# Two fused MLPs behind a small convolution: the low-part products of the narrow output loaded with 64 instead of 128 weight columns

## The reference

```python
# x: (2, 4096, 192), weight: (8, 7): a causal convolution over 7 taps, softmax over the taps, one set per head
w = softmax(weight)                       # 8 heads, 24 channels each
x = sum_k w[h, k] * x_padded[:, s + k, h, :]
x = x.reshape(8192, 192)
h = x @ moe_w_in                          # 192 -> 2048
x = (h * clip(h + 3, 0, 6) / 6) @ moe_w_out   # 2048 -> 192
h = x @ moe2_w_in
x = where(h > 0, h, exp(min(h, 0)) - 1) @ moe2_w_out
```

## Time and profile before

| | |
|---|---|
| time, median of 3 runs | 1122.45 us (1122.15 to 1123.27) |
| the profiled execution's own time | 1123.27 us |
| its span, first to last instruction | 1121.5 us |
| TensorE matmul / weight load busy | 99% / 82% |
| VectorE / ScalarE / GpSimd busy | 80% / 56% / 4% |
| DMA | 22.50 MB, mean 20 GB/s |

### The profile page before, as it was taken

How to read it: one execution, slowest core, us unless ns; L and a number is a source line. 1 busy time by engine, 2 the same in 40 slices (tenths; PEclk the granted TensorE clock), 3 DMA queues, 4 the chain that set the end, 5 groups by cost and what they waited for, 6 DMA issues and landing times.

```text
span 1121.5 us, 24081 instructions
## 1 busy us (share of the span) xinstructions
PE 1115.1 (99%) x9744; PEld 918.0 (82%) x9744; DVE 900.5 (80%) x963; ACT 632.8 (56%) x684; POOL 40.7 (4%) x36
## 2 busy tenths in 40 slices
PE   9999999999999999999999999999999999999998
PEld 6888888888888888888888888888888888888886
DVE  7897887878888788887878878788787887876776
ACT  7665655546555555555555555465555655546554
POOL 4432000000000000000000000000000000000000
PEclk9999999999999999999999999999999999999999
DMA  4310010100101001010010100001000010000000
GB/s 156 119 36 32 1 34 0 33 0 0 33 0 33 0 0 33 0 33 0 0 33 0 33 0 1 32 0 33 0 28 5 0 33 0 14 1 11 6 2 29
DMA packets 14761, 22.50 MB, mean 20 GB/s; under 512 B 1424, under 2 KB 5520, under 8 KB 14736
## 3 DMA queue, kind: packets, MB, share of 16 engines
q1 hardware_dynamic: 14592, 22.12, 6.2%
q10 hardware_dynamic: 144, 0.01, 0.0%
HBM read 15.83 MB, written 6.29 MB: 20 GB/s over the span
## 4 chain that ended last, share of the span: by engine, by line
PE 99%; ACT 0%; DVE 0%; issue 0%; DVEq 0%; ACTq 0%
PE acc_a L691 31%; PE h_ps L677 31%; PE acc_b L699 20%; PE h_ps L684 16%; PE h_ps L841 0%; PE h_ps L832 0%; PE acc_a L832 0%; PE h_ps L707 0%; PE acc_a L762 0%; DVE hidden L525 0%; PE acc_a L739 0%; ACT hidden L343 0%; PE acc_b L756 0%; PE acc_b L747 0%; PE acc_b L741 0%; PE acc_a L746 0%
## 5 line engine op out<-in xcount | busy, mean ns | idle before, releaser
L353 ACT CAST g_hi<-hidden 128x1024 fp32r<-128x1024 f32 x255 | 268.4, 1053 | 352.7 <-DVE hidden L530 238.2
L534 DVE TENSOR_TENSOR g_lo<-hidden,g_hi 128x1024 fp32r<-128x1024 f32 x255 | 313.1, 1228 | 127.9 <-ACT g_hi L353 127.9
L677 PE MATMUL h_ps<-in_hi_a,win_hi_a 64*128 64x512 f32 x1012 | 390.8, 386 | 0.0
L691 PE MATMUL acc_a<-g_hi,wout_hi_a 64*128 64x512 f32 x1012 | 390.8, 386 | 0.0
L677 PE MATMUL h_ps<-in_hi_a,win_lo_a 64*128 64x512 f32 x1012 | 390.7, 386 | 0.0
L691 PE MATMUL acc_a<-g_hi,wout_lo_a 64*128 64x512 f32 x1012 | 390.6, 386 | 0.0
L677 PE MATMUL h_ps<-in_lo_a,win_hi_a 64*128 64x512 f32 x1012 | 390.6, 386 | 0.0
L699 PE MATMUL acc_b<-g_hi,wout_b 64*128 64x512 f32 x1012 | 350.4, 386 | 0.0
L691 PE MATMUL acc_a<-g_lo,wout_hi_a 64*128 64x512 f32 x1012 | 310.1, 386 | 0.0
L699 PE MATMUL acc_b<-g_lo,wout_b 64*128 64x512 f32 x1012 | 310.0, 386 | 0.0
L525 DVE SCALAR_TENSOR_TENSOR hidden<-hidden,h_ps 128x1024 f32<-128x1024 f32 x128 | 156.4, 1222 | 60.9 <-ACT hidden L343 60.8
(11 more groups left out here) (109 smaller groups left out, 1215.5 us busy)
## 6 DMA issues: line engine op xcount, KB each, us to landing
xwin_a<-x_win SPq DMA_DIRECT2D x16, 259.0 KB, 2.7
raw_in<-w_in SPq DMA_DIRECT2D x8, 512.0 KB, 4.0
out_t<-out_a SPq DMA_DIRECT2D x16, 256.0 KB, 2.9
xwin_b<-x_win SPq DMA_DIRECT2D x15, 259.0 KB, 2.9
raw_out<-w_out SPq DMA_DIRECT2D x8, 384.0 KB, 3.7
out_t<-out_b SPq DMA_DIRECT2D x16, 128.0 KB, 2.2
xnext_b<-x_win SPq DMA_DIRECT2D x1, 259.0 KB, 5.9
taps<-tap_w ACTq DMA_DIRECT2D x1, 7.0 KB, 2.7
```

The lines of the kernel that those rows point to most:

```text
L353: nc.scalar.copy(g_hi[:, g % PARTS, :], hidden[:, g % 2, :]).then_inc(hi_ready, 1)
L534: nc.vector.tensor_tensor(g_lo[:, g % PARTS, :], hidden[:, g % 2, :], g_hi[:, g % PARTS, :].bitcast(F32), ALU.subtract).then_inc(lo_ready, 1)
L677: return nc.tensor.matmul(bank(g, c), w[HALVES[r], columns(g, c)], x[HALVES[r], :], start=start, stop=c == 0 and r == 1 and term == 2)
L691: return nc.tensor.matmul(acc_a[acc][:, :], w[HALVES[r], g * CPG + c, :], x[HALVES[r], g % PARTS, c * TOK:(c + 1) * TOK], start=g == 0 and ...
```

## The change

The calls of `out_b_part` with term 1 (the product with `g_lo`) take only the high weights, columns 0 to 63 of `wout_b`, and write only partitions 0 to 63 of the accumulator. Calls with term 0 stay as they are. The product of low weights with low data is no longer computed. The order of the matmuls, the waits, the transfers and the other engines' programs stay the same.

```diff
             def out_b_part(m, g, acc, c, term, r):
-                x = (g_hi, g_lo)[term]
-                return nc.tensor.matmul(acc_b[acc][:, :], wout_b[m][HALVES[r], g * CPG + c, :],
+                x, n = ((g_hi, 2 * DB), (g_lo, DB))[term]
+                return nc.tensor.matmul(acc_b[acc][0:n, :], wout_b[m][HALVES[r], g * CPG + c, 0:n],
                                         x[HALVES[r], g % PARTS, c * TOK:(c + 1) * TOK],
                                         start=g == 0 and c == 0 and term == 0 and r == 1,
                                         stop=g == GROUPS - 1 and c == 1 and term == 0 and r == 0)
```

## The result

The changed kernel takes 1132.6 us (median of 6 runs, 1130.27 to 1132.92), the kernel before 1122.3 us (6 runs, 1121.95 to 1123.27). The ratio over all runs is 1.0085, 95% interval 1.0073 to 1.0098 (the two medians alone give 1.0092). It is slower, by a little under 1%, where no change was forecast.

The account below looks back on a forecast made before the run. TensorE was taken as the bound, its pair step set by streaming 512 tokens. Three terms of 0 us left the profiled 1123.27 us, so the forecast was the median, 1122.4 us, with a range of 1120 to 1237 us.

Parts of the forecast that it names:

- 2: Changed matmuls of `both_products`: 64 columns instead of 128 stream the same 512 tokens, so are not faster; 0 us.
- Step 3: Clusters in `both_products` where 64-column matmuls neighbour 128-column ones: the change of shape drains nothing; 0 us.
- Step 1: Weight loads of 4 of 38 matmuls in `both_products`: 54 ns shorter each, hidden behind the token stream; 0 us.
- rival D: Pairs with narrow loads in `both_products`: loads set the step, so it shrinks; -11 us, 1111 us; chance 0.05.
- A: Two clusters in `both_products`: each change of shape drains the array; +486 us, 1608 us; chance 0.09.
- C: Narrow matmuls in `both_products`: each narrow load is issued late; +114 us, 1236 us; chance 0.10.
- B: Clusters in `both_products`: narrow matmuls do not run beside wide ones of the other half; +229 us, 1352 us; chance 0.05.

Follow-up runs that it names:

- e8: The kernel before, with the narrow products at the very end (L747, L756) widened to 128 columns; ratio 1.0001 to the kernel before.
- e10: All 38 matmuls of `both_products` cut to 96 columns, the rest of every product left out; ratio 1.0177 to the kernel before.
- e9: All 38 matmuls of `both_products` cut to 120 columns, the rest of every product left out; ratio 1.0309 to the kernel before.
- e14: All 38 matmuls of `both_products` cut to 80 columns, the rest of every product left out; ratio 1.0320 to the kernel before.
- e2: The changed kernel with 96 columns instead of 64 in the products with `g_lo`; ratio 1.0116 to the kernel before.
- e6: The changed kernel with 120 columns instead of 64 in the products with `g_lo`; ratio 1.0130 to the kernel before.
- e12: The changed kernel, its narrow products reading columns 64 to 127 of `wout_b` instead of 0 to 63; ratio 1.0077 to the kernel before.
- e1: The changed kernel with narrow `g_lo` products only for rows 64 to 127, the other half wide; ratio 1.0086 to the kernel before.
- e11: The changed kernel, reordered in rows 64 to 127 so that a wide matmul stands between the two narrow ones; ratio 1.0074 to the kernel before.
- e13: All 38 matmuls of `both_products` cut to 112 columns, the rest of every product left out; two profiled executions took 1158.33 and 1137.47 us.

## Why the prediction was wrong

**The step that failed is 2 and 3 together: the row of `second_product`.** Both terms were put at 0 us, and measured together they are +33.3 ns per call, 8.4 us in the span. From 1110.68, 1110.91, 1111.14, 1111.37 the prediction read steps of 0.23 us "into L747 and out of it", found the same from L741 to L746, and took 0 us. All of these were already the uneven steps. 0.23 stands for anything from 225 to 235 ns, and the prediction itself had written that 2.2 ns per changed matmul decide. Over 18 steps, from L740 at 1109.52 to L747 at 1113.67, the same trace gives 4.15 / 18 = 0.2306 us, beside 0.2275 in the earlier trace rows and 0.2266 in the earlier trace rows: some 4 ns per step that stood in the rows and was rounded away. It would not have given the price (in e8 the same 18 steps take 4.13 us, so most of it comes from the start of this stream), but it would have raised the chance of slower.

**Step 1 held in its conclusion on the loads.** A narrow load takes 132 ns (130 forecast) and is worth nothing. The busy time of PEld went up, from 918.0 to 950.6 us, instead of down to 863. It counts the time in which any load runs, and the loads of the two halves overlap less once the halves start apart; added up one by one, the loads of the two traces fell by 52 us (1846.6 to 1794.7), near the 55 forecast. As a sign of step 1 the busy time was a bad choice.

**"The pair's step is set by the streaming of the 512 tokens, which the change leaves alone" was wrong in its second half.** The length of the loads is not the bound, as it said (e10). But the step depends on the number of weight columns, in an order that no sum of durations gives: 226.7 ns at 128, 230.0 at 96, 233.3 at 120 and 80 (e9, e10, e14). One of its two rows was also weaker than it looked. The convolution's pairs of the earlier trace rows stream 256 tokens, not 512:

```profile
8.65 0.38 PE L832 MATMUL acc_a<-xnext_b,diag 64*128 64x256 f32 x1
```

Their 0.216 us shows that two loads fit into less than 0.2266 us. It does not show what a stream of 512 tokens could do, which is how rival D used it.

**Step 3 asked the right question and gave a wrong choice of answers.** A change of shape does not drain (load issued at 500.85, e2 and e6 dearer with 96 and 120 columns than with 64). The Trainium skill, "TensorEngine Tiling (Array Packing)", section Tiling Modes (Key Properties), says "Mode switching requires drain"; the runs show no drain between 128 and 64 columns with the rows unchanged, as the earlier trace rows had it. A row of the trace gives the columns that a matmul uses and not the mode of the array, so whether the narrow matmuls changed the mode at all is not shown.

**The rivals.** A was to cost 0.96 us per cluster and C 0.113 us per narrow matmul with late loads; neither is there. B was to show narrow matmuls alone in their step; they run beside the other half. D was to bring 11 us. None holds; the mechanism, a slower and uneven pace, was on no list. The last sentence of the prediction had it in general ("by however little, since it happens 506 times"), but it blamed shapes that hold each other up between halves, and e8 to e10 show it without that. The range of 1120 to 1237 us contained the time only because C was in it, and C's mechanism is not there: that was luck.

**What stays open.** Why 128 columns keep the even 226.7 ns and the other widths measured do not. The runs exclude the load's duration (e6, e10), a configuration for 64 columns (e2, e9), a difference between neighbours (e9, e10), a second half of the rows (e8) and which 64 columns are read (e12). The width of the load and the width of the matmul go together in one operation and were not told apart. The part of the difference outside the span, about 1.6 us, is open too.

## What to carry to other kernels

Where TensorE is the bound and its matmuls follow each other evenly, an edit to them can change the pace, even one that only takes work away; cutting the weights to fewer columns saved nothing here and cost 0.3 to 3%. Filling the unused columns, even with a product that is not needed, was the faster form. Where two streams share the engine, look at the first calls too: later the slower one sets the length of both, and hides what the other costs by itself (e1, e11). And where a few ns per instruction decide, read a step as an average over many starts, never off two rows of a timeline.

## What was not expected of the hardware

The mean steps lie on a few values. The mean step of a uniform stream was 226.7, 230.0 or 233.3 ns, 3.3 ns apart, with nothing in between in the executions profiled, and one program (e13) was found at two lengths, 1158.33 and 1137.47 us. In the runs with one to three narrow matmuls in a cluster, the extra time per call was 13.3, 20.0, 33.3, 46.7 and 60.0 ns, each within 0.1 ns of a multiple of 6.67. After a narrow matmul, or after the start of `second_product`, a wide stream took two to nine steps to become even again, each up to 9 ns longer than an even one. At the start of `last_product` it was even at once in the kernel before and in e8, and not in the changed kernel. And only the uniform stream of 128 columns was even step by step.
